# Where three engines prepare the weight pieces of the next stage, in an attention kernel on one core

## The reference

```python
# attention: batch 2, 8 heads, 768 positions, head size 64, hash with 6 bits
mask = q_bucket[:, :, :, None] == k_bucket[:, :, None, :]
scores = np.where(mask, scale * np.matmul(q, k.transpose(0, 1, 3, 2)), -1e9)
attn = np.exp(scores - np.max(scores, axis=-1, keepdims=True))
attn = attn / (np.sum(attn, axis=-1, keepdims=True) + 1e-09)
attn_out = np.matmul(attn, v)
# dense layer, 1536 tokens, 512 -> 1024 -> 512
h = x @ w_in
solu = h * softmax(h)
ln = (solu - mean) / np.sqrt(var + 1e-06) * g_ln
x = ln @ w_out
# experts: each token goes to one of 8, 512 -> 1024 -> 512, relu between
```

## Time and profile before

| | us |
|---|---|
| median of 3 runs (786.18 to 789.93) | 787.79 |
| the profiled execution, its time | 788.34 |
| its span, first to last instruction | 786.5 |
| TensorE busy (share of the span) | 628.5 (80%) |
| VectorE busy | 423.3 (54%) |
| ScalarE busy | 323.8 (41%) |
| GpSimd busy | 272.4 (35%) |

### The profile page before, as it was taken

The page is one execution under the profiler, slowest core; times in us unless marked ns, Lnnn a source line. Parts: engine busy times, 40 slices in busy tenths (PEclk is TensorE's granted clock), DMA queues, the critical chain, the costliest instruction groups (busy, mean ns, idle before and its releaser), DMA issues.

```text
span 786.5 us, 12094 instructions
## 1 busy us (share of the span) xinstructions
PE 628.5 (80%) x3574; PEld 508.3 (65%) x3575; DVE 423.3 (54%) x764; ACT 323.8 (41%) x531; POOL 272.4 (35%) x200
## 2 busy tenths in 40 slices
PE   0658686868777787777999999981089999999994
PEld 0446565656565666655888888861078878878883
DVE  2546666666757565714465656546333564646431
ACT  1445555555545455532222222233243455545520
POOL 2365556565656464532123232253400100000010
PEclk9779888898989898987999999995589999999998
DMA  4457834435252515001000000022661756566510
GB/s 132 119 134 210 240 106 96 119 71 143 63 151 56 156 43 135 24 1 70 38 1 0 0 0 0 1 62 112 230 239 43 247 176 206 186 214 211 176 30 26
DMA packets 39262, 83.86 MB, mean 107 GB/s; under 512 B 7485, under 2 KB 10429, under 8 KB 39232
## 3 DMA queue, kind: packets, MB, share of 16 engines
q1 hardware_dynamic: 31952, 72.30, 31.5%
q10 hardware_dynamic: 5040, 4.87, 2.4%
q0 software_dynamic: 2240, 6.31, 2.1%
HBM read 52.09 MB, written 12.35 MB: 82 GB/s over the span
## 4 chain that ended last, share of the span: by engine, by line
PE 61%; DVE 11%; issue 8%; ACT 6%; POOL 5%; SPq 4%; DMA 4%; ACTq 1%; DVEq 1%; POOLq 0%
PE PS L477 8%; PE PS L454 6%; PE PS L464 4%; PE PS L646 4%; PE PS L648 4%; PE PS L647 3%; PE PS L498 3%; PE PS L500 3%; PE PS L627 3%; PE PS L499 3%; PE PS L628 3%; PE PS L629 3%; PE PS L558 3%; PE PS L560 3%; PE PS L559 3%
## 5 line engine op out<-in xcount | busy, mean ns | idle before, releaser
L1223 POOL TENSOR_TENSOR at_P<-at_P,sb_rr 128x768 f32<-128x768 f32 x96 | 138.3, 1468 | 119.2 <-DVE sb_rr L725 119.2
L454 PE MATMUL PS<-at_B,at_A 128*128 128x384 f32 x384 | 105.1, 403 | 35.3 <-DMA at_B<-at_HB 19.0
L712 DVE TENSOR_REDUCE sb_nm<-PS 128x1 f32<-128x768 f32 x96 | 91.6, 954 | 75.2 <-PE PS L454 74.7
L464 PE MATMUL PS<-sb_cst,at_P 128*128 128x128 f32 x576 | 79.5, 286 | 54.3 <-ACT at_PT L1029 54.3
L1017 ACT ACTIVATE at_P<-PS,sb_nb,sb_sc 128x768 f32<-128x768 f32 x96 | 95.7, 1000 | 65.1 <-DVE sb_nb L716 65.1
L454 PEld LDWEIGHTS PS<-at_B,at_A 128*128 128x128 f32 x384 | 72.2, 216 | 57.8 <-ACT at_P L1017 23.6
L464 PEld LDWEIGHTS PS<-sb_cst,at_P 128*128 128x128 f32 x576 | 67.5, 144 | 62.4 <-ACT at_PT L1029 40.2
L941 DVE TENSOR_TENSOR at_W<-at_raw,at_W 128x2048 f32 (+1 forms) x30 | 68.0, 2290 | 70.6 <-ACT at_W L1093 67.9
L1314 POOL DMA_INDIRECT out<-at_yb,sb_to x16 | 15.8, 985 | 204.3 <-DVE at_yb L953 204.3
L1093 ACT ACTIVATE at_W<-at_raw 128x2048 f32 (+1 forms) x32 | 60.4, 1911 | 61.4 <-issue 32.8
L477 PE MATMUL PS<-at_PT,at_V 128*64 128x192 f32 x768 | 85.1, 381 | 0.7 <-DVE at_PT L735 0.7
(11 more groups left out here) (145 smaller groups left out, 1062.8 us busy)
## 6 DMA issues: line engine op xcount, KB each, us to landing
at_raw<-w SPq DMA_DIRECT2D x32, 1024.0 KB, 5.5
at_A<-at_H SPq DMA_DIRECT2D x32, 192.0 KB
at_B<-at_H SPq DMA_DIRECT2D x32, 192.0 KB
rows_by_expert<-at_empty SPq DMA_DIRECT2D x19, 257.0 KB, 6.4
at_XS<-rows_by_expert ACTq DMA_DIRECT2D x17, 256.0 KB, 2.6
at_stg<-w_solu SPq DMA_DIRECT2D x16, 256.0 KB, 3.3
at_R<-qT SPq DMA_DIRECT2D x8, 384.0 KB, 3.3
at_R<-kT SPq DMA_DIRECT2D x8, 384.0 KB, 4.2
```

Of the source, the lines that this page charges most:

```text
L454: m = mm(slot(j)[:, g, :], a[c][:, j * P:(j + 1) * P], b[c][:, g * HALF:(g + 1) * HALF], start=(a is A1), stop=(a is A2))
L464: m = pe.transpose(PS[:, T0 + kt % 3, j * P:(j + 1) * P], Pr[c][w][j][:, kt * P:(kt + 1) * P], ident)
L712: dve.tensor_reduce(nm[:, col], slot(j), AX.XY, ALU.max, negate=True).then_inc(s_nm, 1)
L1223: pool.tensor_tensor(p, p, rr[:, col].broadcast_to([P, S]), ALU.mult).then_inc(s_norm, 1)
```

## The change

Three calls move within `heads`, on three engines. Nothing else changes: the instructions, their operands and their semaphores are the same.

- On VectorE `weights_scaled` comes after the next maximum and after the eviction of kt = 2 of the second half, not before them.
- On ScalarE `weights_high` moves from the place ahead of the evictions of kt = 3 and 4 of the first half to the end of the head's work, after the evictions of the second half and the exponential of head h+2's tile 1. In an odd head it stands just ahead of the high parts of the next q and k.
- On GpSimd `weights_low` comes after the normalisation of head h+1's second half, not between the two. In an odd head it stands just ahead of the low parts of the next q and k.

```diff
--- before.py
+++ after.py
@@ -795,10 +795,10 @@
                     if more:
                         maximum(h + 1, 1 - c, 4)
                     turned(h, 0, 5)
-                    weights_scaled(h, c)
                     if more:
                         maximum(h + 1, 1 - c, 5)
                     turned(h, 1, 2)
+                    weights_scaled(h, c)
                     if left > 0:
                         maximum(h + 2, c, 0)
                     if more:
@@ -1064,7 +1064,6 @@
                     else:
                         act.wait_ge(s_pvev, HEADS // 2)
                         take(0, 0, 0, True)
-                    weights_high(h, c)
                     for kt in (3, 4):
                         turned(h, 0, kt)
                     if more:
@@ -1079,6 +1078,7 @@
                         turned(h, 1, kt)
                     if left > 0:
                         weights_of(h + 2, c, 1)
+                    weights_high(h, c)
                     if c == 1 and left > 1:
                         high_parts(i + 2)
 
@@ -1252,9 +1252,9 @@
                         normalize(h + 1, 1 - c, 0)
                     else:
                         take(0, 0, 0, True)
-                    weights_low(h, c)
                     if more:
                         normalize(h + 1, 1 - c, 1)
+                    weights_low(h, c)
                     if c == 1 and left > 1:
                         low_parts(i + 2)
 
```

## The result

| | before | after |
|---|---|---|
| median of the runs, us | 787.21 | 761.43 |
| ratio, with its 95% interval | | 0.9679 (0.9631 to 0.9727) |
| span of the profiled execution | 786.5 | 760.1 |
| ScalarE stands before L1033 for L729 | 74.6, 16 times | none |
| TensorE stands at L464 for ScalarE's evictions | 54.3, 16 times | none (9.3, 6 times, for VectorE's L735) |

The account below looks back on a forecast made before the run. The start of the fill was taken to bound a pair of heads. Gains of 1.9 + 15.0 + 4.2 + 5.8 = 26.9 us took the profiled 788.34 to 761.4, so a median of 761 was forecast, range 752 to 772.

Parts of the forecast that it names:

- from there (head 4's scores) to the first issue of head 14's fill, five pairs: Fills of heads 6, 8, 10, 12 and 14 each start 3.0 us earlier, 15.0 in all.
- The bound to watch is the start of the fill: Even heads: scores come 9.09 us after the fill's first issue, so only an earlier fill, 3.0 us, counts.
- The even head: Its 4.23 us stall leaves its place; TensorE stands some 6 us in one piece before the scores.
- The odd head: TensorE's 2.91 us stall and the low clock behind it go, 4.3, taken as 4.2; fill 3.0 earlier.
- The second normalisation: GpSimd, odd head: starts at 154.53, 3.0 us earlier, after VectorE's maximum, eviction, rescale, and maximum with inverse.
- The rescale at 0.48: VectorE's L729 at its new place takes 0.48 us, GpSimd being done; upper bound 1.57.
- Rival 1: VectorE's rescale meets GpSimd's normalisation, takes 1.57; five fills and the tail lose 6 × 1.1, 767.5 us; 12%.
- GpSimd's subtraction ahead of the low parts, 1.27: Odd head: 1.27 us of subtraction now precede q and k's low parts, so the fill gains 3.0, not 4.2.
- rival 2: Weight's low part delays the fill if odd heads end no earlier: 1.2 us in each of five pairs, 795; 3%.
- Head 4: Its fill starts 3.0 us earlier but lands into 19 zero-row transfers; scores gain 1.9 (bounds 0 and 3.0).
- that backlog is over only at 92 + 0.34 × 2 = 92.7: Zero-row transfers ahead of head 4's fill end at 92.7, read from DMA shares, so scores start about 93.0.
- The last heads: Heads 13 to 15, no fill behind them: head 13 gains 4.2 us, the tail 5.8 (bounds 4 and 7).

Follow-up runs that it names:

- E7: Changed kernel with the fill's ten issues reordered, only two still waiting for GpSimd's low parts: 719.73 us.
- E8: Kernel before with the fill's ten issues reordered, only two still waiting for GpSimd's low parts: 767.47 us.
- E3: Changed kernel with, in odd heads, high and low parts of q and k ahead of the weight's copy and low part: 756.57 us.
- E2: Changed kernel with VectorE's rescale put back ahead of the maximum of tile 5: 763.61 us.
- E9: Kernel before with the 19 zero-row transfers issued after the last pair's loads: 786.64 us, ratio 0.9997.
- E4: Changed kernel with the 19 zero-row transfers issued after the last pair's loads: 757.91 us.
- E5: Changed kernel with an eleventh issue in each fill, same bytes (the transfer of q's low part split in two): 761.24 us.
- E1: Changed kernel with GpSimd's subtraction put back between the two normalisations: 791.09 us, 1.0044 of before.
- E10: Changed kernel with the fill's issues reordered and the zero-row transfers late: 710.73 us.
- E11: Changed kernel with reordered fill, late zero rows, and q and k's high and low parts ahead of the weight's: 707.87 us, 0.8992 of before.
- E6: Kernel before with an eleventh issue in each fill, same bytes (the transfer of q's low part split in two): 786.25 us, 0.9995 of before.

## Why the prediction was right

The forecast was 761, the measured median 761.43, and the range 752 to 772 held. By its own steps (us of span, from the two traces):

| step of the prediction | forecast | measured |
|---|---|---|
| head 4's scores, from the start of the span | −1.9 | +1.25 (94.90 to 96.15) |
| from there (head 4's scores) to the first issue of head 14's fill, five pairs | −15.0 | −16.4 (195.2 to 178.8) |
| from there to the dense layer's first matmul of tile 1 | −10.0 | −10.7 (80.7 to 69.9) |
| from there to the end | 0 | −0.5 (415.7 to 415.2) |
| all | −26.9 | −26.4 |

The total is closer than its parts: an error of 3.2 us at head 4 stands against 1.4, 0.7 and 0.5 on the other side.

**The bound to watch is the start of the fill: right.** The first issue and the scores stay 9.1 apart in an even head, all that was gained there lies ahead of the first issue, and E7 and E8 move just this. The earlier trace rows names ScalarE's exponential as the releaser of the stall before the scores; E8, which moves only the fill, takes this stall away, so it was the fill.

**The even head: right in its length, not in its parts.** I had some 6 us of standing in one piece. It is 1.58 and 5.19, because VectorE's addition L723 waits for GpSimd's low parts. That delay cost nothing here: in E3, where it is 0.43 and not 1.58, the stall before the scores is still 5.21.

**The odd head: right, a little too small.** A pair gained 3.3 to 3.4, not 3.0. Counted from the even head's scores before (133.87 after, 135.54 before, so 1.67 apart), the copy started at 158.2 in the old time where I had 158.5, because the gain taken for TensorE's path was 4.2 and measured 4.4. The stall and the two terms of the clock added up to 4.3, which is also what the traces have from the scores of tile 5 to the hashes (148.91 to 158.48 before, 147.13 to 152.37 after, 4.3 less); the rest, 0.1, was won ahead of these scores. The second normalisation started at 154.25, where I had 154.53: VectorE came to this place 0.11 sooner, one maximum held its queue for 1.30 and not 1.38, and the rescale holds it for 0.39, not for its 0.48.

**The rescale at 0.48: right.** Rival 1 did not come; E2 shows that even with 1.43 and 1.57 it would have cost 2 us (4 to 5 without its sooner head 4) and not the 6.6 that I gave it, for the subtraction waits for ScalarE's copy in any case. I had that slack in my own numbers (158.85 against 159.3) and did not use it in pricing the rival.

**GpSimd's subtraction ahead of the low parts, 1.27: right in the odd head.** E3 took it away again and brought the low parts 1.17 closer to the normalisation. That it would be worth this much in each pair, which I took for granted in E3 and in rival 2, is not what the runs show: the 4.9 us of E3 came mostly in the first and last heads, and the pairs between gained 0.3, since TensorE's clock stayed lower for longer behind the stall. Rival 2 rested on the same price, but its condition, an odd head that ends no earlier, did not hold.

**Head 4: wrong.** The step that failed is "that backlog is over only at 92 + 0.34 × 2 = 92.7", from which I had the scores at 93.0. The shares of 1.00 and 0.34 do not show the end of the zero rows. The trace lists the DMA packets, and their size tells the transfer: 2056 bytes are a zero row, 3072 a row of q or k. In the kernel before the last zero-row packet starts at 88.7, so what fills 90 to 92 is the fill itself. E9, without zero rows, has a low share at the end of its fill too (0.21 in 90 to 92).

In the changed kernel the last zero-row packet starts at 89.3. The fill's first packet of q and k starts at 86.6 in both kernels, which is 1.2 us behind the first issue in the kernel before and 4.0 us in the changed one (1.2 in E4, with no zero rows under way). So the fill that was issued 2.8 us sooner stood behind the zero rows and its data moved no sooner: nothing was to be gained, not 1.9. The idea of a backlog was right, and its end was misread. The zero rows do not end at the same time in every run: in E2 their last packet starts at 86.4, and head 4's scores begin at 93.19 there.

Why the scores came 1.25 us later than before, and not at the same time, is not shown. The whole fill was issued by 91.4, but its packets of q and k last to 94 or so (92.9 before), the share stayed at 0.85 and above to 96, and transfers issued behind it (92.24 and 92.78) ran meanwhile. The scores came 5.5 us behind the start of the last issue instead of 2.1. No run moved these later transfers away.

**The last heads: right** within 0.7: the stall of 2.24 is gone, and the dense layer's twelve matmuls from 331.01 run at the full clock.

**What I had wrong of the fill itself** did not touch the sum, which used its 9.09 us as a whole: I took it for ten issues in a row, and E5 shows that an eleventh costs nothing.

## What to carry to other kernels

A preparation that nobody waits for soon should not stand in an in-order queue ahead of work that somebody waits for, and when it is moved, the parts that wait for it on other engines have to move with it: here the copy and the rescale, without the subtraction, made the kernel slower than before (E1), while the rescale's own place was worth only 2 us (E2). Before a stall is priced as won, look for the next release on the same engine, here a transfer whose start did not move as far as the stall was long. And then ask which parts of that transfer really need the last input: on top of the change, sending eight of ten early was worth more than the change itself (41.7 us to 26), and without it 19.7.

## What the runs showed of the hardware that I had not expected

- A VectorE addition of 128 x 3 numbers in SBUF took 0.16 to 0.17 us with GpSimd idle. While GpSimd subtracted two SBUF operands (the low parts) it took 0.84 (kernel before, 166.39), 1.47 (changed kernel and E10) and 0.29 (E11). In all four it ended 0.03 us behind GpSimd's low parts. So it did not run slower in proportion to its work: it lasted until GpSimd was done.
- A single stall of 2.91 us in a busy stretch was followed by the lower clock: the granted clock of the kernel before is 1.00 in 148 to 152, 0.85 in 153 to 154 and 0.50 in 154 to 156. In E7, where no stall from 130 to 260 is longer than 1.6 us, it stays at 1.00.
- Eleven issues on SyncE's queue took the same 7.70 us as ten with the same bytes (E5).
- Transfers issued on SyncE's queue behind 19 blocks of zeros moved their first rows of q and k only 1.4 to 2.6 us before the last zero-row packet started, in the kernel before, the changed kernel, E2, E3, E5 and E6, and the first of them had been issued 3 to 7 us before that packet.
